# Transposes of the attention probabilities as products with a diagonal matrix of reciprocals, and a rearranged opening

## The chip, the cores and the metric

The kernel runs on one core of one Trainium2 chip. The metric is device time in microseconds (us) of one execution; the median of several is given. Engines work from their own queues, each strictly in the order the program gives it: PE (matrix products), DVE and POOL (elementwise), ACT (copies and functions) and SP (which issues most transfers). They wait for each other through semaphores, written s_... and m_... here.

## The reference

```python
scores = scale * np.matmul(q, k.transpose(0, 1, 3, 2))          # 4 batches, 8 heads, 576 x 64
kth = np.partition(scores, -top_k, axis=-1)[..., -top_k:-top_k + 1]   # top_k = 32
scores = np.where(scores >= kth, scores, -1000000000.0)
attn = np.exp(scores - np.max(scores, axis=-1, keepdims=True))
attn = attn / (np.sum(attn, axis=-1, keepdims=True) + 1e-09)
x = np.matmul(attn, v)                                          # heads side by side: 576 x 512
gate = 1.0 / (1.0 + np.exp(-causal_conv5(x, conv_w)))
x = (gate * (x @ w_val)) @ w_out
u = x + np.real(np.fft.fft(np.fft.fft(x, axis=1), axis=2))
un = (u - u.mean(-1)) / np.sqrt(u.var(-1) + 1e-06)
out = u + np.maximum(un @ w_ch1, 0.0) @ w_ch2
```

## The kernel before

All engines walk through one list of **slots**. Slot s starts the attention tile s (128 query rows against 576 keys of one head; 9 tiles make a pair of heads, 36 a batch, 144 all). The tile t then travels through later slots: scores on PE and their copy `s_sb` on ACT in slot t; the selection of the 32 largest on DVE (`top`, four MAX8 and three MATCH_REPLACE8 for each tile, two tiles at a time) in slots t+1 to t+3; the two bias values on POOL (L917, L918) and the exponent on ACT (`prob`, L655 and L660, with the row sum in `psum_row`) in slot t+5; five 128x128 transposes of `prob` on PE (L455, into `p_t`) and their copy `pT` on ACT (L668) in slot t+6; the product with `v` (L471, `attend`) in slot t+7, for two tiles together, so in five of nine slots.

The softmax is normalised at the end. DVE computes `rinv`, the reciprocal of the row sum (`reciprocal`, L801 and L803); at the end of `attend` two more products (L475) of the broadcast `rinv` with the identity put the reciprocals beside the result; ACT copies both halves to `or_sb` (L677), and POOL multiplies them into `x_new` (L929), which the next stage reads.

From slot 43 on each slot also holds one to three **steps** of the gated layer and the feed-forward layer of the batch before (`val`, `zed`, `seq`, `proj`, `trn`, `ch0`, `ch1`). They are laid out by a table of costs in `steps_by_slot`. A `ch0` or `ch1` step is `hidden` on PE (L574), two copies on ACT (L716, L717), their difference `hid_lo` on POOL (L982) and, one step later, `sums` on PE (L588). In a slot PE does the scores, the transposes, the first step, `attend`, then the other steps. ACT does copy of scores, copy of `pT`, exponent, weight part, first step, output copy, other steps. POOL does the biases, the weight part, the first step, `scale_out` (L929), the other steps. In slots 2 to 33 ACT and POOL also split one weight tile into a high and a low part for each slot (L686 on ACT, then L934 on POOL). After the last attention tile the steps of the fourth batch run alone.

At the start SP issues the loads of q and k of the first pair (first head to `q_raw`, `k_raw`, second head to `z`), then v, the identity, 2.8 MB of tables, two weight tiles, and in slot 0 the q and k of the second pair. ACT takes the high parts of q and k (`high_queries`, `high_keys`), POOL and DVE the low parts (`split_low`). At the ends of slots 0 and 1 ACT takes the high parts of q and k of the next pair.

The products in 32-bit floats show two records each in the trace (a high and a low pass), a transpose one; the f32r products of the scores and of the feed-forward layer show one.

## Time and profile before

| | |
|---|---|
| median of 3 runs | 1178.61 us (1178.06 to 1179.55) |
| profiled execution | 1173.26 us, of which 1171.5 us are its span |
| busy share of the span | PE 88%, DVE 75%, ACT 53%, POOL 34% |
| granted TensorE clock, mean | 0.948 of full speed |

The profiled execution is 5 us below the median. The views used are the busy time by stretches of the span, the timeline (instructions in order of time with the idle time of the engine ahead of each, and who ended it), the groups by line, and the answer by tile. In the timeline, several instructions of one kind that follow each other are one row, with their count after the x; the time of such a row is from the first start to the last end.

### The profile page before, as it was taken

To read this page: it belongs to the slowest core of one execution; us is meant where nothing else is said; L and a number is where in the kernel's file an instruction comes from. 1 tells how busy PE (TensorE), PEld (TensorE's weight loads), DVE (VectorE), ACT (ScalarE), POOL (GpSimd) and SP (SyncE) were. 2 spreads that over 40 slices of the span, in tenths; PEclk is the share of its full clock that TensorE was granted. 3 is DMA by queue.
4 is the path that set the end of the run, shared out by engine and by line. 5 is a ranking of instruction groups with operands and counts; after the bars stand their busy time and mean duration, and the time that the engine had idled before them with its cause. 6 is when DMAs were issued, how large, how long until landed. Compare 5 with 4: busy or idle time off the path is not lost.

```text
span 1171.5 us, 19830 instructions
## 1 busy us (share of the span) xinstructions
PE 1036.1 (88%) x6608; PEld 827.8 (71%) x6608; DVE 872.8 (75%) x1900; ACT 617.6 (53%) x1253; POOL 404.1 (34%) x704
## 2 busy tenths in 40 slices
PE   2776675589988999999989999999889999999998
PEld 1445554466667888866578888875678888648887
DVE  3999999998998897897898987897988960320000
ACT  2676675645466665645466756455565654012211
POOL 1443552223344422332443423233443222233221
PEclk9986566789999999999999999999999999999999
DMA  6755456111256675620367675411367555207974
GB/s 199 228 178 174 156 189 231 32 31 57 68 172 227 246 257 208 205 67 21 112 222 253 251 231 199 145 57 59 134 204 259 201 211 196 99 1 288 343 269 164
DMA packets 81188, 200.37 MB, mean 171 GB/s; under 512 B 8384, under 2 KB 26560, under 8 KB 81088
## 3 DMA queue, kind: packets, MB, share of 16 engines
q1 hardware_dynamic: 81088, 199.11, 50.2%
q8 instruction: 54, 0.88, 0.3%
q14 instruction: 46, 0.38, 0.1%
HBM read 177.58 MB, written 21.50 MB: 170 GB/s over the span
## 4 chain that ended last, share of the span: by engine, by line
PE 38%; issue 26%; DVE 18%; POOL 12%; ACT 3%; SPq 1%; DMA 1%; POOLq 0%; DVEq 0%; ACTq 0%
PE p_m L482 11%; PE p_m L588 10%; PE p_m L574 10%; DVE rest L770 8%; DVE top L776 6%; POOL hid_lo L982 3%; PE p_t L455 2%; PE p_t L471 2%; POOL bias L918 2%; PE p_s L442 2%; POOL bias L917 2%; DVE top L761 1%; ACT prob L655 1%; POOL x_new L929 1%; POOL gate L941 1%
## 5 line engine op out<-in xcount | busy, mean ns | idle before, releaser
L776 DVE MAX8 top<-rest 128x8 f32<-128x576 f32 x432 | 304.6, 746 | 0.0
L770 DVE MATCH_REPLACE8 rest<-top,rest 128x576 f32<-128x576 f32 x288 | 211.7, 743 | 0.0
L982 POOL TENSOR_TENSOR hid_lo<-hid,hid_hi 128x256 fp32r<-128x256 f32 (+1 forms) x128 | 105.0, 820 | 302.5 <-ACT hid_hi L717 302.5
L588 PE MATMUL p_m<-w_st,hid_hi 128*128 128x512 f32 x640 | 202.3, 397 | 1.5 <-POOL hid_lo L982 1.5
L574 PE MATMUL p_m<-un_hi,w_st 128*128 128x320 f32 (+1 forms) x1024 | 165.6, 304 | 13.3 <-ACT hid_hi L717 9.5
L655 ACT ACTIVATE prob<-s_sb,bias 128x576 f32<-128x576 f32 x144 | 111.1, 771 | 104.3 <-POOL bias L918 104.0
L574 PEld LDWEIGHTS p_m<-un_hi,w_st 128*128 128x128 f32 x1024 | 142.8, 189 | 26.4 <-issue 23.4
L455 PE MATMUL p_t<-id_sb,prob 128*128 128x128 f32 x720 | 118.3, 299 | 45.1 <-ACT prob L660 23.7
L471 PE MATMUL p_t<-pT,v_sb 128*64 128x128 f32 (+1 forms) x1600 | 111.8, 293 | 38.2 <-issue 26.1
L648 ACT ACTIVATE s_sb<-p_s 128x576 f32<-128x576 f32 x144 | 93.2, 647 | 96.2 <-PE p_s L442 96.0
L442 PE MATMUL p_s<-k_hi,q_st 128*128 128x512 f32 (+1 forms) x320 | 116.1, 365 | 29.7 <-ACT s_sb L648 19.9
L471 PEld LDWEIGHTS p_t<-pT,v_sb 128*64 128x64 f32 x1600 | 92.2, 153 | 67.1 <-issue 50.7
L588 PEld LDWEIGHTS p_m<-w_st,hid_hi 128*128 128x128 f32 x640 | 113.4, 189 | 20.7 <-POOL hid_lo L982 3.0
L588 PE MATMUL p_m<-w_st,hid_lo 128*128 128x512 f32 x320 | 127.0, 397 | 0.0
L716 ACT ACTIVATE hid<-p_m 128x256 f32<-128x256 f32 (+1 forms) x128 | 51.5, 403 | 139.7 <-PE p_m L574 139.7
L660 ACT ACTIVATE prob<-prob,bias 128x576 f32<-128x576 f32 x144 | 111.8, 776 | 13.1 <-ACT prob L655 0.4
L455 PEld LDWEIGHTS p_t<-id_sb,prob 128*128 128x128 f32 x720 | 82.6, 149 | 50.1 <-ACT prob L660 44.4
L761 DVE MAX8 top<-s_sb 128x8 f32<-128x576 f32 x144 | 101.4, 744 | 11.9 <-ACT s_sb L648 11.9
L668 ACT ACTIVATE pT<-p_t 128x640 f32<-128x640 f32 x144 | 101.4, 704 | 14.8 <-PE p_t L455 14.7
L770 DVE MATCH_REPLACE8 rest<-top,s_sb 128x576 f32<-128x576 f32 x144 | 105.7, 741 | 0.0
L442 PEld LDWEIGHTS p_s<-k_hi,q_st 128*128 128x128 f32 x320 | 66.8, 209 | 53.8 <-issue 29.7
L853 DVE TENSOR_TENSOR u<-p_m,u 128x512 f32<-128x512 f32 (+1 forms) x20 | 12.6, 681 | 112.9 <-PE p_m L588 112.9
(83 smaller groups left out, 1580.1 us busy)
## 6 DMA issues: line engine op xcount, KB each, us to landing
w_st<-w_split SPq DMA_DIRECT2D x256, 512.0 KB, 4.5
w_split<-w_st SPq DMA_DIRECT2D x32, 512.0 KB, 3.0
q_raw<-qT SPq DMA_DIRECT2D x62, 144.0 KB, 2.9
k_raw<-kT SPq DMA_DIRECT2D x62, 144.0 KB, 3.0
u<-w_ch SPq DMA_DIRECT2D x32, 256.0 KB, 3.4
v_sb<-v SPq DMA_DIRECT2D x16, 256.0 KB, 3.6
wslot<-w_val SPq DMA_DIRECT2D x4, 1024.0 KB, 5.3
wslot<-w_out SPq DMA_DIRECT2D x4, 1024.0 KB, 5.3
```

What stands on the lines that cost most here:

```text
L442: mm = pe.matmul(p_s[:, k0:k1], q_st[h][p % 2][:, cols], k[:, k0:k1], start=n == 0, stop=n == len(parts) - 1)
L455: mm = pe.transpose(p_t[:, c * P:c * P + P], prob[t % 3][:, c * P:c * P + P], id_sb[:, :])
L471: pe.matmul(p_o[D * h:D * h + D, 0, 0:n], v_sb[p % 2][:, c, D * h:D * h + D], pT[tt % 3][:, c, c0:c0 + n], start=c == 0, stop=c == NCH - 1 ...
L482: mm = pe.matmul(bank[0:m, c0:c1], a, w, start=k == 0, stop=k == len(lhs) - 1, skip_group_check=True)
L574: mm = pe.matmul(mbank(HIDDEN_BANK[g], n), w1_st[i % NB1][:, w, k, :], x[:, k, at:at + n], start=part + k == 0, stop=part + k == KC + 1)
L588: mm = pe.matmul(mbank(j), h[i % 2][:, P * j:P * j + P], w2_st[i % NB2][:, w, :], start=f == 0 and part == 0, stop=f == FC - 1 and part == 2)
L655: act.activation(prob[t % 3][:, 0:S], s_sb[t % NS][:, :], ACT.Prelu, bias=bias[t % NK][:, 1:2], scale=-BIG, alpha=1.0 / BIG).then_inc(s_dr ...
L660: act.activation(prob[t % 3][:, 0:S], prob[t % 3][:, 0:S], ACT.Exp, bias=bias[t % NK][:, 0:1], scale=-SCALE, accum_out=psum_row[:, t % NK: ...
L761: dve.max(top[tt % NK][:, 0:8], s_sb[tt % NS][:, :]).then_inc(s_chain, 1)
L770: dve.match_replace(rest[tt % 2][:, :], top[tt % NK][:, 8 * n - 8:8 * n], src[:, :], LOWEST).then_inc(s_chain, 1)
L776: found = dve.max(top[tt % NK][:, 8 * n:8 * n + 8], rest[tt % 2][:, :])
L982: pool.tensor_tensor(hid_lo[i % 2][:, 0:WIDTH[g]], hid[:, 0:WIDTH[g]], hid_hi[i % 2][:, 0:WIDTH[g]].bitcast(F32), ALU.subtract).then_inc(m ...
```

## The change

- `normaliser` on POOL takes the place of `reciprocal` on DVE and of `scale_out`. For each tile, in the slot of its exponent and behind the first step, POOL adds to the row sum, raises to the power -1, and multiplies the identity by the result: `norm`, a 128x128 matrix with the reciprocals on its diagonal (two buffers).
- `transpose_p` is a 32-bit product of `prob` with `norm` instead of a transpose with the identity. It waits for `s_norm` instead of `s_exp`.
- `attend` loses its two products with `rinv`; `store_out` on ACT copies 128 columns straight to `x_new`.
- Opening: the four loads of the first head are issued by SP (k) and ACT (q) instead of SP alone; the loads of the second pair come ahead of the tables; the low part of the first k is taken by DVE instead of POOL; and for the second pair the high parts of q and k of the first head are taken at the ends of slots 2 and 3 (before 0 and 1), the low ones at the end of slot 3 (before 2).

```diff
 def transpose_p(t):
-    pe.wait_ge(s_exp, t + 1)
-    if t == 0:
-        pe.wait_ge(s_const, 16)
-    else:
+    pe.wait_ge(s_norm, t + 1)
+    if t:
         pe.wait_ge(s_pT, t)
     if t and unit_due(t + TRANSPOSE - 1):
-        pe.wait_ge(s_or, unit_of(t + TRANSPOSE - 1 - ATTEND) + 1)
+        pe.wait_ge(s_x, unit_of(t + TRANSPOSE - 1 - ATTEND) + 1)
     for c in range(NCH):
-        mm = pe.transpose(p_t[:, c * P:c * P + P], prob[t % 3][:, c * P:c * P + P], id_sb[:, :])
+        mm = pe.matmul(p_t[:, c * P:c * P + P], prob[t % 3][:, c * P:c * P + P], norm[t % 2][:, :],
+                       start=True, stop=True)
...
-    for h, (tt, c0) in enumerate(src):
-        mm = pe.matmul(p_o[D * h:D * h + D, 1, 0:n],
-                       rinv[:, tt % NK:tt % NK + 1].broadcast_to((P, D)),
-                       id_sb[:, c0:c0 + n], start=True, stop=True, skip_group_check=True)
...
-    act.activation(or_sb[n_u % 2][:, :, 0:n], p_o[:, :, 0:n], ACT.Copy).then_inc(s_or, 1)
+    act.activation(x_new[p % NX][:, at:at + n], p_o[:, 0:n], ACT.Copy).then_inc(s_x, 1)
...
-    dve.tensor_scalar(rinv[:, c], psum_row[:, c], EPS_SUM, 2.0, ALU.add, ALU.mult).then_inc(s_radd, 1)
-    dve.wait_ge(s_radd, t // 2 + 1)
-    dve.reciprocal(rinv[:, c], rinv[:, c]).then_inc(s_rinv, 1)
...
-HIGH_Q, HIGH_K, LOW = {0: 0, 4: 1}, {1: 0, 5: 1}, {2: 0, 6: 1}
+HIGH_Q0, HIGH_K0, LOW0 = {2: 0, 5: 1}, {3: 0, 5: 1}, {3: 0, 6: 1}
...
+def normaliser(t):
+    c = slice(t % NK, t % NK + 1)
+    pool.wait_ge(s_exp, t + 1)
+    pool.tensor_scalar(rinv[:, c], psum_row[:, c], EPS_SUM, 2.0, ALU.add, ALU.mult).then_inc(s_radd, 1)
+    pool.wait_ge(s_radd, t + 1)
+    pool.tensor_tensor(rinv[:, c], rinv[:, c], power[:, 1:2], ALU.pow).then_inc(s_rinv, 1)
+    pool.wait_ge(s_rinv, t + 1)
+    if t == 0:
+        pool.wait_ge(s_const, 16)
+    elif t >= 2:
+        pool.wait_ge(s_tr, t - 1)
+    pool.tensor_scalar(norm[t % 2][:, :], id_sb[:, :], rinv[:, c], None, ALU.mult).then_inc(s_norm, 1)
...
-    if unit_due(s):
-        scale_out(s - ATTEND)
+    if due(s, EXPONENT):
+        normaliser(s - EXPONENT)
```

POOL in the first batch, slots 8 and 9, before (`w_st` is the low part of a weight tile):

```order
L917 TENSOR_SCALAR bias<-top 128x1 [waits s_topk]
L918 TENSOR_SCALAR bias<-top 128x1
L934 TENSOR_TENSOR w_st<-u,w_st 128x512 [waits s_whi]
L929 TENSOR_TENSOR x_new<-or_sb 128x128 [waits s_or]
L917 TENSOR_SCALAR bias<-top 128x1 [waits s_topk]
L918 TENSOR_SCALAR bias<-top 128x1
L934 TENSOR_TENSOR w_st<-u,w_st 128x512 [waits s_whi]
```

The same two slots on POOL in the changed kernel:

```order
L916 TENSOR_SCALAR bias<-top 128x1 [waits s_topk]
L917 TENSOR_SCALAR bias<-top 128x1
L935 TENSOR_TENSOR w_st<-u,w_st 128x512 [waits s_whi]
L922 TENSOR_SCALAR rinv<-psum_row 128x1 [waits s_exp]
L924 TENSOR_TENSOR rinv<-rinv,power 128x1 [waits s_radd]
L930 TENSOR_SCALAR norm<-id_sb,rinv 128x128 [waits s_tr,s_rinv]
L916 TENSOR_SCALAR bias<-top 128x1 [waits s_topk]
L917 TENSOR_SCALAR bias<-top 128x1
L935 TENSOR_TENSOR w_st<-u,w_st 128x512 [waits s_whi]
L922 TENSOR_SCALAR rinv<-psum_row 128x1 [waits s_exp]
L924 TENSOR_TENSOR rinv<-rinv,power 128x1 [waits s_radd]
L930 TENSOR_SCALAR norm<-id_sb,rinv 128x128 [waits s_tr,s_rinv]
```

The multiplication of the output is gone, and in every slot three instructions stand behind the weight part that make `norm`.

PE at the end of slot 8 and the start of slot 9, before (one row of L471 stands for ten products of `attend`):

```order
L471 MATMUL p_t<-pT,v_sb 64x128 [waits s_v_in0,s_rinv,s_pT]
L471 MATMUL p_t<-pT,v_sb 64x128 x9
L475 MATMUL p_t<-id_sb,rinv 64x128 x2
L442 MATMUL p_s<-k_hi,q_st 128x512 [waits s_copy,s_lo0]
L442 MATMUL p_s<-k_lo,q_st 128x512
L442 MATMUL p_s<-k_hi,q_st 128x64
L442 MATMUL p_s<-k_lo,q_st 128x64
L455 MATMUL p_t<-id_sb,prob 128x128 [waits s_or,s_pT,s_exp]
L455 MATMUL p_t<-id_sb,prob 128x128 x4
```

The same place on PE in the changed kernel:

```order
L478 MATMUL p_t<-pT,v_sb 64x128 [waits s_v_in0,s_pT]
L478 MATMUL p_t<-pT,v_sb 64x128 x9
L451 MATMUL p_s<-k_hi,q_st 128x512 [waits s_copy,s_lo0]
L451 MATMUL p_s<-k_lo,q_st 128x512
L451 MATMUL p_s<-k_hi,q_st 128x64
L451 MATMUL p_s<-k_lo,q_st 128x64
L462 MATMUL p_t<-norm,prob 128x128 [waits s_x,s_pT,s_norm]
L462 MATMUL p_t<-norm,prob 128x128 x4
```

Two products have left `attend`, and the wait at the head of the transposes is now for POOL's `s_norm`, with `s_x` in the place of `s_or`.

ACT in the opening, slots 0 to 3, before:

```order
L642 ACTIVATE k_hi<-z 128x576 [waits s_qk_in1]
L648 ACTIVATE s_sb<-p_s 128x576 [waits s_qk]
L635 ACTIVATE q_st<-q_raw 128x576 [waits s_qk_in0]
L648 ACTIVATE s_sb<-p_s 128x576 [waits s_qk]
L642 ACTIVATE k_hi<-k_raw 128x576 [waits s_qk_in0]
L648 ACTIVATE s_sb<-p_s 128x576 [waits s_qk]
L686 ACTIVATE w_st<-u 128x512 [waits s_wraw0]
L648 ACTIVATE s_sb<-p_s 128x576 [waits s_qk]
```

The same place on ACT in the changed kernel:

```order
L645 ACTIVATE k_hi<-z 128x576 [waits s_qk_in1]
L651 ACTIVATE s_sb<-p_s 128x576 [waits s_qk] x3
L691 ACTIVATE w_st<-u 128x512 [waits s_wraw0]
L638 ACTIVATE q_st<-q_raw 128x576 [waits s_qk_in0]
L651 ACTIVATE s_sb<-p_s 128x576 [waits s_qk]
L691 ACTIVATE w_st<-u 128x512 [waits s_wraw1]
L645 ACTIVATE k_hi<-k_raw 128x576 [waits s_qk_in0]
```

Three copies of scores now come ahead of the first instruction that waits for a transfer of the second pair or of a weight tile.

## Rows read from the trace of the kernel before

**Rows 1.** Busy time by stretches (us, instructions in brackets), granted clock, transfers.

```profile
core 0: us, PE busy (x) PEld busy (x) DVE busy (x) ACT busy (x) POOL busy (x), PEclk, DMA share, GB/s
40.00:76.00 36.00, 30.20 (x170) 18.61 (x169) 35.90 (x80) 27.18 (x51) 16.29 (x26) 1.00 0.63 195
76.00:220.00 144.00, 92.43 (x581) 76.93 (x579) 143.34 (x305) 96.32 (x181) 56.77 (x95) 0.66 0.52 170
220.00:271.00 51.00, 38.44 (x258) 31.19 (x259) 50.76 (x114) 27.02 (x51) 12.01 (x27) 0.90 0.12 31
271.00:523.00 252.00, 242.35 (x1653) 195.90 (x1651) 219.64 (x475) 149.86 (x309) 92.55 (x167) 1.00 0.52 175
775.00:998.00 223.00, 214.30 (x1459) 171.90 (x1457) 164.30 (x358) 122.43 (x256) 76.19 (x144) 0.98 0.49 171
```

**Rows 2.** Timeline of the opening: start, duration, engine, line, tiles, [idle before].

```profile
16.13 0.60 SPq L324 DMA_DIRECT2D k_raw<-kT  x1
22.47 0.68 ACT L635 ACTIVATE q_st<-q_raw 128x576 fp32r<-128x576 f32 x1 [10.50 <-DMA k_raw<-kT]
23.72 0.76 DVE L761 MAX8 top<-s_sb 128x8 f32<-128x576 f32 x1 [10.96 <-ACT s_sb L648]
39.43 5.40 PE L482 MATMUL p_m<-gv,gate 128*128 128x512 f32 x8
```

**Rows 3.** Timeline, first batch: POOL's weight parts of slots 5, 33; slot 11 whole.

```profile
38.86 1.28 POOL L934 TENSOR_TENSOR w_st<-u,w_st 128x512 fp32r<-128x512 f32 x1 [4.46 <-ACT w_st L686]
...
189.21 1.29 POOL L934 TENSOR_TENSOR w_st<-u,w_st 128x512 fp32r<-128x512 f32 x1 [3.79 <-ACT w_st L686]
...
64.91 0.70 ACT L668 ACTIVATE pT<-p_t 128x640 f32<-128x640 f32 x1
65.52 0.77 ACT L655 ACTIVATE prob<-s_sb,bias 128x576 f32<-128x576 f32 x1
66.32 0.77 ACT L660 ACTIVATE prob<-prob,bias 128x576 f32<-128x576 f32 x1
67.00 0.19 ACT L660 ACTIVATION_READ_ACCUMULATOR prob<-prob,bias 128x1 f32 x1
...
67.79 1.28 POOL L934 TENSOR_TENSOR w_st<-u,w_st 128x512 fp32r<-128x512 f32 x1 [2.64 <-ACT w_st L686]
67.24 0.76 PE L455 MATMUL p_t<-id_sb,prob 128*128 128x128 f32 x5 [1.23 <-ACT prob L660]
```

**Rows 4.** Timeline of POOL at 296 and 302 us: small operations and a 128x128 product.

```profile
296.03 0.22 POOL L958 TENSOR_SCALAR rstd<-mv 128x1 f32<-128x1 f32 x1 [3.15 <-DVE mv L838]
296.34 0.58 POOL L960 TENSOR_TENSOR rstd<-rstd,power 128x1 f32<-128x1 f32 x1
297.00 0.24 POOL L917 TENSOR_SCALAR bias<-top 128x1 f32<-128x1 f32 x1
...
302.80 0.46 POOL L929 TENSOR_TENSOR x_new<-or_sb 128x128 f32<-128x128 f32 x1
```

**Rows 5.** Timeline of PE: transposes, products of several widths, at full clock.

```profile
280.85 3.62 PE L482 MATMUL p_m<-wfeat,gate 128*128 128x257 f32 x16
284.40 1.31 PE L471 MATMUL p_t<-pT,v_sb 128*64 128x128 f32 x20
285.54 0.39 PE L475 MATMUL p_t<-id_sb,rinv 128*64 128x128 f32 x4
285.86 0.50 PE L442 MATMUL p_s<-k_hi,q_st 128*128 128x512 f32 x1
...
641.79 0.77 PE L455 MATMUL p_t<-id_sb,prob 128*128 128x128 f32 x5
642.31 1.19 PE L574 MATMUL p_m<-un_hi,w_st 128*128 128x256 f32 x8
```

**Rows 6.** Timeline of PE: the transposes at the lower clock.

```profile
156.10 1.33 PE L455 MATMUL p_t<-id_sb,prob 128*128 128x128 f32 x5 [1.87 <-ACT prob L660]
```

**Rows 7.** Timeline of POOL and PE around one `ch1` step and one `proj` step.

```profile
704.41 0.88 POOL L982 TENSOR_TENSOR hid_lo<-hid,hid_hi 128x320 fp32r<-128x320 f32 x1 [2.84 <-ACT hid_hi L717]
705.63 0.77 PE L455 MATMUL p_t<-id_sb,prob 128*128 128x128 f32 x5
...
566.09 0.76 PE L455 MATMUL p_t<-id_sb,prob 128*128 128x128 f32 x5
569.33 0.57 POOL L960 TENSOR_TENSOR rstd<-rstd,power 128x1 f32<-128x1 f32 x1
```

**Rows 8.** Groups by line and shape: count, busy us, mean ns.

```profile
L801 DVE TENSOR_SCALAR rinv<-psum_row 128x2 f32<-128x2 f32 x72 | 12.7, 177 | 78.4 <-ACT prob L660 78.4
L803 DVE RECIPROCAL rinv<-rinv 128x2 f32<-128x2 f32 x72 | 11.9, 166 | 2.5
L677 ACT ACTIVATE or_sb<-p_t 128x256 f32<-128x256 f32 x64 | 24.3, 380 | 68.1 <-PE p_t L475 68.1
L907 POOL TENSOR_TENSOR q_st<-q_raw,q_st 64x576 fp32r<-64x576 f32 x16 | 22.6, 1410 | 6.6 <-ACT k_hi L642 6.6
L909 POOL TENSOR_TENSOR k_lo<-k_raw,k_hi 128x576 fp32r<-128x576 f32 x16 | 24.2, 1516 | 0.0
```

**Rows 9.** The page's part on transfers: count, KB each, us to landing.

```profile
u<-w_ch SPq DMA_DIRECT2D x32, 256.0 KB, 3.4
```

99 lines of the change are left out of this document (46 added, 53 removed).

## The prediction

> **What bounds the kernel now.** I read the busy time by stretches first [rows 1]. It shows three regimes. From 40 to 271 us, the attention of the first batch, DVE is busy for 99% of the time (143.34 of 144 us in the middle stretch) while PE has 64% there at a granted clock of 0.66, a mix of its two levels, 1.2 and 2.4 GHz. From 271 to 998 us PE is the bound: 242.35 of 252 us in one batch period at full clock, DVE 87%. From 998 us on the feed-forward steps of the last batch run alone (174 us) and nothing in the change touches them.
>
> The timeline of the opening comes second [rows 2]. The last load of the second pair is issued at 16.13 us and lands at 22.47; ACT waits for it for 10.50 us with the copy of the second tile's scores queued behind, and DVE idles 10.96 us. Third, the timeline of one slot of the first batch [rows 3] shows which steps follow each other between two transposes, and fourth the PE rows [rows 5, 6] give the price of a transpose and of its neighbours.
>
> **What becomes a loop.** Before, the transposes of tile t in slot t+6 waited for the exponent of slot t+5. Now they wait for POOL's `norm`, and POOL makes it only after the weight part of that slot, which itself waits for ACT's weight copy, which stands behind the exponent. The exponent of the next tile stands on ACT behind the copy `pT` of these transposes. So transposes, `pT`, exponent, ACT weight copy, POOL weight part, `norm`, next transposes are one closed chain per slot. Its length, link by link:
>
> - `pT` start to the end of the exponent: 64.91 to 67.19, 2.28 us; from there to the end of POOL's weight part (67.79 + 1.28 = 69.07): 1.88 us [rows 3].
> - `norm`: the trace of before has no such group, its parts have neighbours [rows 4]. The first small operation to the start of the power is 0.31 us (296.03 to 296.34), the power to the next operation 0.54 to 0.66, and a 128x128 product 0.46. Together 1.37 us. The last is one input and a scalar per row instead of two inputs, so 0.24 (a small operation) to 0.46; I take 0.46, since its size is that of the product. Bounds 1.1 to 1.5.
> - transposes to `pT`: 0.80 us in all at full clock now, 1.36 at the lower one [rows 5, 6].
>
> What a product costs instead of a transpose has two ends. Five transposes take 0.52 us from their start to the next group (641.79 to 642.31), 0.104 each. A 32-bit product with 257 columns takes (284.40 - 280.85)/16 = 0.222 us for each of its two records; scaled to 128 columns 0.111, so 0.222 for a product and 1.11 for five. The other end is `attend`: (285.54 - 284.40)/20 = 0.057 a record, 0.57 for five [rows 5]. In `attend` two products of 64 output rows each stand side by side in different halves of the array, here a product fills it, so I take 1.11, that is +0.59 us per tile at full clock. At the lower clock the five take 1.33 in the row, ten records some 2.4, +1.07 (my estimate: 0.21 a record added to the last one's 0.27 doubled).
>
> On its rule about this the Trainium skill ("TensorE: Matmul & The Clock Gate", Terms) says that the transpose mode is four times faster for 32-bit floats. By that a product would be 0.42 us, five 2.08, and the 106 tiles below would add 165 us instead of 63. The row above speaks for about two times.
>
> The chain is then 0.80 + 0.54 (0.59 less overlap at the tail) + 2.28 + 1.88 + 1.37 + 0.04 for the semaphore = 6.9 us at full clock, and 0.56 + 0.55 more = 8.0 at the lower.
>
> **The sum, part by part** (made against the profiled execution, 1173.26 us).
>
> *Opening.* DVE could start its selection some 10.6 us earlier, nearly the 10.96 us. But ACT then waits for the first weight tile, which lands with the tables at about 22 us (now they are all in flight until 22.47), and POOL reaches its first weight parts only then. Its part is done at 22.5 + 0.6 + 1.28 = 24.4, the third weight tile is requested only then and lands 3.4 us later [rows 9], its copy and part end near 30 behind the split of q and k (2.9 [rows 8]); biases, exponent (2.3 with `pT`, 1.6 without) and the part of slot 5 (1.9 [rows 3]) follow: 34 instead of 40.14. **-6** (0 to -11, DVE's whole idle time).
>
> *First batch, slots 5 to 33.* POOL's weight parts end at 38.86 + 1.28 = 40.14 in slot 5 and at 189.21 + 1.29 = 190.50 in slot 33 [rows 3]: 150.4 us for 28 slots, 5.37 each. That is DVE's pace. The chain is longer, so it takes over. The first 7 slots ran at full clock, 7 x 6.9 = 48. For the other 21 I keep the clock of the stretch, 0.66, so a third at full clock: 0.33 x 6.9 + 0.67 x 8.0 = 7.6, times 21 = 160. In three of these slots POOL also splits q and k (1.41 + 1.52 [rows 8]) between `norm` and the next biases, about 1 us each that nothing covers: 3. Together 211 against 150: **+61**. At full clock throughout and with `norm` at 1.1: 28 x 6.6 = 185, +35; at the lower clock throughout with 1.5: +75. What DVE saves (0.177 + 0.166 us for two tiles [rows 8]) buys nothing here, since DVE now waits.
>
> *Slots 34 to 42.* No weight parts, so the chain is 1.9 us shorter, 5.0 to 6.1, against 5.7 now (51 us for nine slots [rows 1]). DVE is caught up by then. **-2** (-7 to +4).
>
> *PE work from slot 43 on.* 106 tiles still have their transposes here: 106 x 0.59 = +63. Each of 60 `attend` groups loses its last products, 285.54 to 285.86 = 0.32 [rows 5]: -19. Together **+44** (-13 with the price of `attend`). PE is 96% busy, so nearly all of it lands on the path; of the 4% idle I let 5 us cover some: **-5**.
>
> *Waits for `norm` from slot 43 on.* In each slot I compared the time at which POOL has done its first step (and ACT its exponent) with the start of the transposes in the next slot, and took as late what is missing to the 1.37 us of `norm`. Two of the pairs are in [rows 7]: after a `ch1` step `hid_lo` ends at 704.41 + 0.88 = 705.29 and the transposes start at 705.63, 0.34 later, so they would be 1.0 us late; after `proj` POOL ends at 569.90 while the transposes had started at 566.09, 5.2 late. In the period from 523 us this gives, for 20 of 36 slots: nine slots with one feed-forward step in front 0.6 to 1.8 each, 10 in all; three slots with `val` 5.6; seven with `seq`, `proj` or `trn` 15.8. That is 31 for a period, 92 for three. PE only hides it where a slot has a second step (late 0 in twelve of these). In the second kind POOL's own date hangs on DVE, which will have more room: after `proj` the true lateness is the chain from PE's last product over DVE's four operations and POOL's two to `norm`, less what PE has to do meanwhile, 2 to 3 us instead of 3 to 5. That takes off 8 a period, 24. POOL's split of q and k behind `norm` adds about 1.2 in two slots a period, 7. Together **+75** (35, if half of it goes into slack, to 110).
>
> *Nothing:* ACT's shorter output copy (0.380 us for 256 columns [rows 8]) and POOL's lost multiplication (0.46 [rows 4]) lie in slack of engines 53% and 34% busy. The tables start some 2 to 3 us later (four transfers stand ahead of them); before, the last transfer of the opening had landed at 22.47 and PE first read them at 39.43 [rows 2].
>
> Sum: -6 + 61 - 2 + 44 - 5 + 75 = +167. The profiled execution would be 1340, and against the median, 1178.6 + 167, **1346 us**.
>
> **The rivals.**
>
> *The waits vanish in the later batches.* If most of the later slots have slack that the single rows don't show, only the first batch's chain and PE's work remain, with 10 us of waits: 1281. For it: POOL is 34% busy. Against it: the hand-over after a lone step has 0.3 us of room and recurs in every period.
>
> *The clock stays up in the first batch.* The granted clock fell to 0.66 where PE had transposes and short products with gaps between. With products instead the stretch could keep 2.4 GHz: 21 x (7.6 - 6.9) = 15 less, 1331. Against it: PE's share per slot falls, as slots get longer. The Trainium skill (same page, Part 4: PE-mode transpose) says that transposes don't count as activity for the clock; that rule is what this case would follow, and no row of before separates it from the gaps.
>
> *A product costs four transposes.* Then 106 x (1.56 - 0.59) = 103 more: 1449.
>
> *`norm` never comes last at all, but the work stays.* Opening and PE's work alone: 1178.6 - 6 + 39 = 1212. Against it stands the closed chain.
>
> *Faster than before.* The mechanism is POOL running ahead: `norm` is ready before PE asks for it in every slot, DVE's pace is kept in the first batch, and a product costs what `attend` shows. Price: -11 in the opening, -6 for DVE's 36 reciprocals and sums (18 x 0.34), -13 on PE: 1149. It decides at the end of POOL's first step: `norm` would have to fit in the 0.34 us of room [rows 7], and in the first batch in less than nothing, since the weight part ends at 69.07, 1.8 us after the transposes started at 67.24 [rows 3]. It is the least likely.
>
> **How the numbers follow.** Forecast 0.62 (own range 1300 to 1395); waits vanish later 0.13; clock 0.12; four times the price 0.04; no wait at all 0.05; faster 0.03; no change 0.01. The range 1270 to 1400 takes in the first three and their bounds and leaves out about 0.15. A measurement of this kernel tells some 0.2% from no change. Faster 0.03, within 0.2% 0.01, slower 0.96.
>
> **What the profile would show.** In the first batch DVE's busy share falls from 99% to some 70 to 75%, its idle time ends with ACT's copies of scores, and POOL's weight parts come 7 to 8 us apart. PE's idle time before the transposes ends with POOL's `norm`, in nearly every slot of the first batch and in about half of the later ones. The group of transposes has 1440 records, ten in a row 1.1 to 1.2 us long. A period of the middle grows from 252 to about 290 us; the part after the last tile stays at 174. Wrong would be: DVE still at 99% in the first batch (no closed chain), a period under 265 (waits were hidden), ten records under 0.7 us (price of `attend`), or a clock near 1.00 between slots 13 and 33.

## The result and the profile after

The changed kernel takes **1422.55 us** (median of 4 executions, 1419.65 to 1426.52), the kernel before 1178.34 beside it. The ratio is 1.208, with a 95% interval of 1.205 to 1.211: 21% slower. The prediction was 1346 with a range of 1270 to 1400. The sign and the two mechanisms (a closed chain in the first batch, more work and waits for PE later) were right, the size was not: 167 us were forecast and 244 came. The largest step that failed is a term that the prediction put at nothing, the lower clock of PE's work behind its waits in the later periods.

The busy time by stretches of the changed kernel: the slots 6 to 33, 34 to 42, and two periods of 36 slots. The stretches end at the starts of the copies `pT`, so that they hold the same slots as those of other kernels below.

```profile
core 0: us, PE busy (x) PEld busy (x) DVE busy (x) ACT busy (x) POOL busy (x), PEclk, DMA share, GB/s
44.00:281.50 237.50, 145.04 (x737) 117.65 (x737) 152.82 (x305) 108.35 (x204) 102.46 (x174) 0.63 0.35 112
281.50:338.70 57.20, 38.95 (x232) 34.22 (x231) 43.23 (x87) 29.85 (x56) 21.86 (x47) 0.68 0.31 97
338.70:641.40 302.70, 269.57 (x1745) 221.06 (x1745) 208.12 (x425) 149.54 (x304) 132.95 (x255) 0.97 0.42 139
641.40:945.10 303.70, 269.55 (x1745) 220.91 (x1745) 213.25 (x436) 149.40 (x304) 133.46 (x255) 0.97 0.42 142
```

The kernel before, in the same slots of the first batch and in its second period:

```profile
core 0: us, PE busy (x) PEld busy (x) DVE busy (x) ACT busy (x) POOL busy (x), PEclk, DMA share, GB/s
40.00:194.00 154.00, 108.56 (x659) 83.77 (x658) 153.38 (x331) 109.25 (x205) 68.30 (x108) 0.72 0.55 176
496.50:748.80 252.30, 243.02 (x1645) 195.42 (x1645) 218.26 (x471) 148.49 (x306) 92.52 (x168) 0.99 0.50 171
```

In the first batch DVE's share has fallen from 99% [rows 1] to 64%, and nothing else has risen to take its place: no engine is the bound there, a chain is. In the periods PE is still busiest, but it is busy for 27 us more and idle for 34 us instead of 9, and its granted clock is 0.97 instead of 0.99.

One turn of the chain in the first batch, from the timelines of PE, ACT and POOL of the changed kernel (columns as in [rows 2]):

```profile
158.27 2.50 PE L462 MATMUL p_t<-norm,prob 128*128 128x128 f32 x10 [1.86 <-POOL norm L930]
160.80 0.71 ACT L671 ACTIVATE pT<-p_t 128x640 f32<-128x640 f32 x1 [3.72 <-PE p_t L462]
161.40 0.77 ACT L658 ACTIVATE prob<-s_sb,bias 128x576 f32<-128x576 f32 x1
162.26 0.78 ACT L663 ACTIVATE prob<-prob,bias 128x576 f32<-128x576 f32 x1
162.94 0.19 ACT L663 ACTIVATION_READ_ACCUMULATOR prob<-prob,bias 128x1 f32 x1
...
163.73 1.26 POOL L935 TENSOR_TENSOR w_st<-u,w_st 128x512 fp32r<-128x512 f32 x1 [4.82 <-ACT w_st L691]
165.08 0.19 POOL L922 TENSOR_SCALAR rinv<-psum_row 128x1 f32<-128x1 f32 x1
165.35 0.57 POOL L924 TENSOR_TENSOR rinv<-rinv,power 128x1 f32<-128x1 f32 x1
166.03 0.63 POOL L930 TENSOR_SCALAR norm<-id_sb,rinv 128x128 f32<-128x128 f32 x1
...
166.71 1.65 PE L462 MATMUL p_t<-norm,prob 128*128 128x128 f32 x6 [5.06 <-POOL norm L930]
```

Every row waits for the one above it. The products take 2.53 us until `pT` starts, `pT` and the exponent 2.33 (to 163.13), the weight copy and the weight part 1.86 (to 164.99), `norm` 1.67 (to 166.66), and 0.05 us later the next products start: 8.44 us. In the stretch 44 to 281.5, 18 of the 28 slots are 8.3 to 8.6 us long; the mean is 8.49.

Two groups of the page: the products and the multiplication that makes `norm` (the last figures are busy us, mean ns, and idle time before with its releaser).

```profile
L462 PE MATMUL p_t<-norm,prob 128*128 128x128 f32 x1440 | 239.3, 323 | 201.5 <-POOL norm L930 201.5
...
L930 POOL TENSOR_SCALAR norm<-id_sb,rinv 128x128 f32<-128x128 f32 x144 | 94.2, 654 | 14.9
```

PE waits 201.5 us for `norm` in the whole span. In the period from 641.4 to 945.1 it is 31.7 us in 20 waits, from the view of waits of that stretch:

```profile
PE p_t L462 <- POOL norm L930: 31.7, 20, 4.8
```

The table compares stages of the profiled executions (before, this one is 5 us below its median) by the starts of the `pT` copies of tiles 0, 28, 37, 73, 109 and 143 in the timelines, in us (forecast: the prediction's terms, those of slots 43 on divided by three).

| stage | before | after | more | forecast |
|---|---|---|---|---|
| until slot 6 | 39.8 | 44.0 | +4.2 | -6 |
| slots 6 to 33 | 153.8 | 237.6 | +83.8 | +61 |
| slots 34 to 42 | 48.8 | 57.2 | +8.4 | -2 |
| slots 43 to 78 | 254.1 | 302.7 | +48.6 | +38 |
| slots 79 to 114 | 252.3 | 303.7 | +51.4 | +38 |
| slots 115 to 148 | 235.3 | 284.6 | +49.3 | +38 |
| the rest | 187.4 | 188.1 | +0.7 | 0 |
| span | 1171.5 | 1417.8 | +246.3 | +167 |

### The profile page after: what moved, and what is told of

Same layout as the page of the kernel before. It is cut to its first block, busy times and chain, and to the rows that moved or that the text cites. A ratio compares the mean times of both kernels' runs of the same rounds, so it can differ in the third digit from the quotient of the medians.

```text
span 1417.8 us, 20820 instructions
## 1 busy us (share of the span) xinstructions
PE 1163.5 (82%) x7008; PEld 948.0 (67%) x7008; DVE 855.7 (60%) x1758; ACT 619.6 (44%) x1253; POOL 571.0 (40%) x1055
## 4 chain that ended last, share of the span: by engine, by line
PE 55%; POOL 19%; ACT 10%; issue 10%; DVE 4%; DMA 1%; SPq 1%; POOLq 0%; ACTq 0%; DVEq 0%
PE p_t L462 15%; PE p_m L485 14%; PE p_m L577 10%; PE p_m L591 10%; ACT prob L658 4%; POOL norm L930 4%; POOL rinv L924 4%; PE p_t L478 3%; POOL w_st L935 2%; PE p_s L451 2%; POOL hid_lo L983 2%; ACT prob L663 2%; POOL rinv L922 2%; ACT w_st L691 1%; DVE rest L777 1%
## 5 line engine op out<-in xcount | busy, mean ns | idle before, releaser
L462 PE MATMUL p_t<-norm,prob 128*128 128x128 f32 x1440 | 239.3, 323 | 201.5 <-POOL norm L930 201.5
L462 PEld LDWEIGHTS p_t<-norm,prob 128*128 128x128 f32 x1440 | 209.4, 227 | 213.1 <-POOL norm L930 213.0
L671 ACT ACTIVATE pT<-p_t 128x640 f32<-128x640 f32 x144 | 101.4, 704 | 303.7 <-PE p_t L462 303.7
L768 DVE MAX8 top<-s_sb 128x8 f32<-128x576 f32 x144 | 105.1, 749 | 184.0 <-ACT s_sb L651 184.0
L577 PE MATMUL p_m<-un_hi,w_st 128*128 128x320 f32 (+1 forms) x1024 | 173.1, 313 | 7.6 <-issue 3.8
L577 PEld LDWEIGHTS p_m<-un_hi,w_st 128*128 128x128 f32 x1024 | 150.1, 198 | 19.7 <-issue 16.5
L591 PEld LDWEIGHTS p_m<-w_st,hid_hi 128*128 128x128 f32 x640 | 114.2, 190 | 18.9 <-POOL hid_lo L983 1.1
L930 POOL TENSOR_SCALAR norm<-id_sb,rinv 128x128 f32<-128x128 f32 x144 | 94.2, 654 | 14.9
```

Source lines behind the costliest of these rows:

```text
L462: mm = pe.matmul(p_t[:, c * P:c * P + P], prob[t % 3][:, c * P:c * P + P], norm[t % 2][:, :], start=True, stop=True)
L577: mm = pe.matmul(mbank(HIDDEN_BANK[g], n), w1_st[i % NB1][:, w, k, :], x[:, k, at:at + n], start=part + k == 0, stop=part + k == KC + 1)
L591: mm = pe.matmul(mbank(j), h[i % 2][:, P * j:P * j + P], w2_st[i % NB2][:, w, :], start=f == 0 and part == 0, stop=f == FC - 1 and part == 2)
L930: pool.tensor_scalar(norm[t % 2][:, :], id_sb[:, :], rinv[:, c], None, ALU.mult).then_inc(s_norm, 1)
```

## Experiments

My theory from these rows: the time goes into a closed chain over PE, ACT and POOL, whose price is set by `norm` standing behind late work on POOL; a second, smaller part is PE's own work; and the clock adds to both, because PE pauses before each group of products. The rivals: the products themselves are the cost, or POOL's operations are too long. The stages of all kernels, measured as above, by tiles (in `later`, `ahead`, `shift` and `relief`, whose transposes come one slot later, the same tiles lie one slot further on):

| kernel | slots 6-33 | 34-42 | 43-78 | 79-114 | 115-148 | clock, whole span |
|---|---|---|---|---|---|---|
| before | 153.8 | 48.8 | 254.1 | 252.3 | 235.3 | 0.948 |
| after | 237.6 | 57.2 | 302.7 | 303.7 | 284.6 | 0.902 |
| `opening` | 151.7 | 49.3 | 255.1 | 252.2 | 235.3 | 0.948 |
| `product` | 155.7 | 48.2 | 271.5 | 266.7 | 249.0 | 0.967 |
| `wait` | 209.7 | 50.6 | 288.1 | 298.5 | 272.6 | 0.886 |
| `later` | 182.7 | 47.4 | 276.0 | 279.7 | 255.7 | 0.939 |
| `ahead` | 145.5 | 39.6 | 278.1 | 266.5 | 244.4 | 0.972 |
| `early` | 181.3 | 58.2 | 273.4 | 272.7 | 252.5 | 0.951 |
| `one` | 208.1 | 47.1 | 280.6 | 283.3 | 264.8 | 0.930 |
| `warm` | 227.2 | 57.9 | 302.8 | 303.8 | 284.5 | 0.933 |
| `shift` | 146.8 | 49.8 | 271.6 | 260.2 | 241.0 | 0.939 |
| `relief` | 144.2 | 47.7 | 266.7 | 261.7 | 239.5 | 0.937 |
| `lighten` | 146.1 | 48.2 | 251.8 | 252.0 | 233.3 | 0.955 |

### The opening alone

```diff
-                load_qk(0, 0)
+                for half in range(2):
+                    sp.dma_start(k_raw[D * half:D * half + D, :], kT[0, 0]).then_inc(s_qk_in[0], 16)
...
+                load_qk(1, 0)
...
+HIGH_Q0, HIGH_K0, LOW0 = {2: 0, 5: 1}, {3: 0, 5: 1}, {3: 0, 6: 1}
```

> The kernel before with the opening of the change alone; transposes, reciprocals and output as before. Theory (DVE sets the pace of the first batch, so what it no longer idles at the start is gained): the second tile's selection starts at 13.4 us instead of 23.7, later stalls at the first weight tile give some 2 us back, so 8 us less, 1170 us (0.993). Rival (the wait of 7.6 us that ACT now has for the first weight tile moves the stall and keeps it): within 3 us of before.

Measured: 1171.59 us, ratio 0.9953 (0.9936 to 0.9969), 5.7 us less. The total is near the expected 1170, though the gain is not where I put it: in its trace the copy `pT` of tile 0 starts at 39.03 instead of 39.78, not 8 us earlier. The two profiled executions differ by only 1.2 us (spans of 1170.3 and 1171.5), so the traces don't show where the other 4.5 of the 5.7 us lie. Where the gain of the opening was lost shows in the opening of the changed kernel, whose part up to the exponent is the same (timelines of DVE, ACT, SP's queue, POOL and PE):

```profile
13.37 0.76 DVE L768 MAX8 top<-s_sb 128x8 f32<-128x576 f32 x1 [1.59 <-ACT s_sb L651]
...
32.68 0.43 SPq L351 DMA_DIRECT2D u<-w_ch  x1
...
36.84 0.63 ACT L691 ACTIVATE w_st<-u 128x512 fp32r<-128x512 f32 x1 [2.47 <-DMA u<-w_ch]
...
37.55 1.27 POOL L935 TENSOR_TENSOR w_st<-u,w_st 128x512 fp32r<-128x512 f32 x1 [4.89 <-ACT w_st L691]
...
41.45 2.50 PE L462 MATMUL p_t<-norm,prob 128*128 128x128 f32 x10 [8.73 <-POOL norm L930]
```

DVE selects from the second tile at 13.37 instead of 23.72 [rows 2], 10.4 us earlier. But the weight part of slot 5 ends at 38.82 instead of 40.14, only 1.3 us earlier: its tile is requested at 32.68, because SP had four loads and a store that waits for POOL ahead of it. In the changed kernel the first products then wait for `norm` until 41.45.

### The product alone

```diff
-        mm = pe.transpose(p_t[:, c * P:c * P + P], prob[t % 3][:, c * P:c * P + P], id_sb[:, :])
+        mm = pe.matmul(p_t[:, c * P:c * P + P], prob[t % 3][:, c * P:c * P + P], id_sb[:, :],
+                       start=True, stop=True)
```

> The kernel before with the five transposes of each tile written as 32-bit products with the identity, same waits, same result. It prices the product alone. Theory (a product costs two records of 0.11 us, nearly all of it on the path from slot 43 on, nothing in the first batch where DVE is the bound): 106 tiles x 0.6 = 64 us more, 1242 us, clock of the first batch not above 0.7. Rival 1 (a product costs four transposes): 165 us more, 1343. Rival 2 (products count as activity for the clock where transposes don't): granted clock of 76 to 220 us near 1.0 instead of 0.66.

Measured: 1223.54 us, ratio 1.040 (1.038 to 1.042), 46 us more. The price of a product, from its timeline and its stretches:

```profile
606.67 1.36 PE L455 MATMUL p_t<-id_sb,prob 128*128 128x128 f32 x10
607.79 1.18 PE L575 MATMUL p_m<-un_hi,w_st 128*128 128x256 f32 x8
```

```profile
43.00:198.60 155.60, 113.53 (x798) 92.70 (x797) 154.77 (x330) 109.36 (x205) 70.00 (x106) 0.84 0.53 169
518.20:784.90 266.70, 261.94 (x1826) 216.55 (x1825) 220.09 (x472) 151.11 (x304) 91.10 (x167) 1.00 0.48 161
```

Ten records take 1.12 us to the next group, against 0.52 for five transposes [rows 5]: +0.60, where the prediction took 0.59. The rival of four times the price is refuted. A period grows by 14.4 us: PE is busy 18.9 longer (36 tiles x 0.52), and 4.5 of that falls into idle time. In the first batch, where DVE is the bound, the products cost nothing (1.9 us in 28 slots). And the granted clock there is 0.84 instead of 0.72, with the same pace. In slots 34 to 42 it is 0.79 in both kernels. How much it varies by itself shows in `opening`, whose PE work is the same as before: 0.76 and 0.68 in these two stretches.

### The wait alone

```diff
-        mm = pe.matmul(p_t[:, c * P:c * P + P], prob[t % 3][:, c * P:c * P + P], norm[t % 2][:, :],
-                       start=True, stop=True)
+        mm = pe.transpose(p_t[:, c * P:c * P + P], prob[t % 3][:, c * P:c * P + P], id_sb[:, :])
```

(against the changed kernel; the transposes still wait for `norm`, but don't use it)

> The changed kernel with the five products turned back into transposes with the identity, which still wait for POOL's norm; the normalisation is left out of the result. It prices the closed chain alone. Theory (the chain over POOL makes most of the loss, and its length is the sum of its links): in the first batch about 7.2 us a slot at the lower clock instead of 8.45, 50 us more than before from slot 6 to slot 34; in each later period 20 to 30 us of waits for norm; together 1178 - 8 + 50 + 80 - 19 = 1280 us. Rival (the product makes the loss, the wait only takes what PE idles anyway): under 1220 us.

Measured: 1350.46 us, ratio 1.148 (1.145 to 1.150). That is 173 us more than before and 70 over what I expected, so the wait is dearer than forecast. Its stretches, slots 6 to 33 and the second period:

```profile
42.40:252.10 209.70, 117.95 (x597) 88.18 (x597) 152.29 (x307) 108.03 (x205) 101.79 (x174) 0.60 0.39 125
590.80:889.30 298.50, 257.02 (x1565) 204.10 (x1564) 215.56 (x435) 148.79 (x305) 136.49 (x255) 0.93 0.43 144
```

In the period this kernel has *less* work on PE than the one before (the products with `rinv` are gone, 1565 records instead of 1645), and PE is yet busy for 257.0 us instead of 243.0: the same work runs at a granted clock of 0.93 instead of 0.99. With products in the place of the transposes and the same waits the clock is 0.97, and the period only 5 us longer (303.7). So in this period the two parts don't add up: with the waits in place, the product's 14 us are for the greater part offset by a better clock. The other two periods don't repeat this. There the clock of `wait` is 0.96 and 0.94, that of the changed kernel 0.97 and 0.96, and the products cost 14.6 and 12.0 us (302.7 against 288.1, 284.6 against 272.6). In the first batch, where the chain is closed, the products do cost: 237.6 against 209.7, 1.0 us a slot.

### One slot more between the exponent and the products

```diff
-SELECT, EXPONENT, TRANSPOSE, ATTEND = 1, 5, 6, 7
+SELECT, EXPONENT, TRANSPOSE, ATTEND = 1, 5, 7, 8
```

> The changed kernel with the transposes and the product with v one slot later (7 and 8 slots behind the scores instead of 6 and 7); same operations, same result. The exponent then no longer stands behind the transposes of the tile before it, so the chain is open. Theory (it is the chain, not POOL's load): slots of the first batch back to 5.4 us, no waits for norm above a few us a period, what stays is PE's work: 1178 - 8 + 5 for one more slot + 3 x 18 = 1229 us. Rival (POOL is too busy with 1.7 us more a slot): first batch still above 7 us a slot, over 1320 us.

Measured: 1273.84 us, ratio 1.082 (1.080 to 1.084). The chain over PE is open, 149 us come back, but the first batch needs 182.7 us, 6.5 a slot, and not DVE's 5.4. The timelines of POOL and ACT show what closes instead:

```profile
124.25 0.30 POOL L917 TENSOR_SCALAR bias<-top 128x1 f32<-128x1 f32 x1
124.58 0.78 ACT L658 ACTIVATE prob<-s_sb,bias 128x576 f32<-128x576 f32 x1 [1.12 <-POOL bias L917]
...
126.92 1.27 POOL L935 TENSOR_TENSOR w_st<-u,w_st 128x512 fp32r<-128x512 f32 x1 [2.37 <-ACT w_st L691]
...
129.23 0.63 POOL L930 TENSOR_SCALAR norm<-id_sb,rinv 128x128 f32<-128x128 f32 x1
...
130.26 0.30 POOL L917 TENSOR_SCALAR bias<-top 128x1 f32<-128x1 f32 x1
```

Biases, exponent, weight copy, weight part, `norm`, next biases: 6.0 us in this turn, all on ACT and POOL; the copies `pT` come 3.3 to 8.7 us apart in that stretch, so it is not closed in each of them, and that this loop sets the mean of 6.5 is shown only by the next experiment. `norm` stands at the end of POOL's slot and ahead of the next biases, so it lengthens this loop too. I had not seen it; before, it was 1.7 us shorter and hidden behind DVE.

### And `norm` right behind the biases

```diff
                     if due(s, EXPONENT):
                         biases(s - EXPONENT)
+                    if due(s, EXPONENT + 1):
+                        normaliser(s - EXPONENT - 1)
```

(on top of the last edit, with the old call removed)

> As the kernel with the transposes one slot later, and POOL makes norm of the tile before directly behind the biases, where it no longer waits for ACT's exponent and runs beside it. Theory (with the chain over PE open, the first batch hangs on a second chain, biases, exponent, weight copy, weight part, norm, next biases, 6.0 us; without norm in it 4.4): first batch back to DVE's pace, 5.4 to 5.6 us a slot, 1274 - 28 x 1.0 = 1246, and less in the later periods, where the step behind norm starts sooner: 1220 to 1246 us. Rival (POOL's load, not its place in the chain): first batch stays at 6.5 us a slot, 1270 us.

Measured: 1209.07 us, ratio 1.027 (1.025 to 1.029).

```profile
43.80:189.30 145.50, 104.61 (x734) 86.73 (x734) 145.36 (x296) 105.56 (x203) 104.74 (x179) 0.85 0.60 194
507.00:773.50 266.50, 257.95 (x1746) 212.49 (x1746) 212.20 (x435) 148.85 (x305) 133.64 (x255) 1.00 0.48 162
```

DVE is the bound again (145.36 of 145.5 us), and the second period is that of the product alone (266.5 against 266.7; the first is 6.5 us longer, the third 4.6 shorter). It issues the same operations as the changed kernel, POOL's among them, and is 213 us faster. It is 31 us slower than the kernel before, 48 if its gain of 17 us in slots 6 to 42 is left aside. So POOL's load and the products together explain at most some 50 of the 244 us: the rest is where `norm` stands and the slot of room behind it, which this run changes together. The second row also bears on the price of the clock. The changed kernel does the same work in its period in 269.55 us instead of 257.95, 11.6 us more, at 0.97 instead of 1.00. Not all of it is the clock: `early` below has the slots of the changed kernel and a clock of 1.00, and its PE is busy for 260.01 us, 2.1 more than here.

### `norm` ahead of the weight part and the first step

```diff
+                    if due(s, EXPONENT):
+                        normaliser(s - EXPONENT)
                     if part_due(s) is not None:
                         split_weights(part_due(s))
```

(transposes in their old slot, the old call removed)

> The changed kernel with norm made on POOL ahead of the weight part and of the first step, transposes in their slot. Theory (the chain stays closed but loses POOL's weight part or step): first batch 8.45 - 1.87 = 6.6 us a slot at the lower clock, 28 x 1.9 = 52 us less, and most of the 32 us of waits in each later period gone: 1422 - 52 - 3 x 25 = 1295 us. Rival (POOL's order does not matter, only its load): within 20 us of 1422.

Measured: 1265.16 us, ratio 1.074 (1.072 to 1.076), 30 less than expected. In the first batch the chain is still closed, without the weight part: 6.5 us a slot, 2.0 less than before that edit, about the 1.86 of that link. In the second period, from its stretches and its waits:

```profile
551.80:824.50 272.70, 260.01 (x1746) 213.24 (x1745) 216.06 (x435) 149.60 (x305) 135.46 (x255) 1.00 0.47 158
```

```profile
PE p_t L462 <- POOL norm L930: 6.7, 7, 2.1
```

The waits for `norm` fall from 31.7 to 6.7 us, 25 less, but the period is 31 shorter: PE's idle time falls by 21.5 us in all, and with the clock back at 1.00 PE is busy for **9.5 us** less. This is what I had missed in my expectation as in the prediction: a microsecond of waiting removed here brings 1.2 back.

### `norm` from one operation

```diff
-                    pool.tensor_scalar(rinv[:, c], psum_row[:, c], EPS_SUM, 2.0, ALU.add, ALU.mult).then_inc(s_radd, 1)
-                    pool.wait_ge(s_radd, t + 1)
-                    pool.tensor_tensor(rinv[:, c], rinv[:, c], power[:, 1:2], ALU.pow).then_inc(s_rinv, 1)
-                    pool.wait_ge(s_rinv, t + 1)
...
-                    pool.tensor_scalar(norm[t % 2][:, :], id_sb[:, :], rinv[:, c], None, ALU.mult).then_inc(s_norm, 1)
+                    pool.tensor_scalar(norm[t % 2][:, :], id_sb[:, :], psum_row[:, c], None, ALU.mult).then_inc(s_norm, 1)
```

(the kernel leaves out the reciprocal, so its output is not normalised; ACT's wait for the sum becomes a wait for `norm`)

> The changed kernel with the sum and the power left out: norm is the identity times the row sum in one operation, so the result is not normalised. 0.95 us less on POOL for each tile. Theory (each microsecond of norm lies on the path wherever PE waits for it: all 37 slots of the first batch, 19 of 36 in each period): 37 x 0.95 + 3 x 19 x 0.95 x 0.8 = 35 + 43, 1422 - 78 = 1344 us. Rival (the semaphore hand-overs and the order make the loss, not the length): under 30 us less.

Measured: 1317.04 us, ratio 1.118 (1.116 to 1.120). The chain row by row loses 165.08 to 166.03, 0.95 us; the slots 6 to 33 lose 29.5 / 28 = 1.05. In the first batch the chain's length is thus the time, link for link. The second period loses 20.4: its waits for `norm` fall from 31.7 us in 20 places to 15.0 in 11, and PE is busy for 264.49 us instead of 269.55, at 0.98. The last part, 5.1 us, is as in the last experiment, and with the other periods it is a reason why the gain of 106 us was above the expected 79.

### Filler products against the clock

```diff
+                    if 14 <= s < 42:
+                        fill(s, 5)
                     if due(s, TRANSPOSE):
                         transpose_p(s - TRANSPOSE)
```

(five products of 128x512 into an unused part of `p_m`, between the scores and the transposes, in the changed kernel)

> The changed kernel with five more 512-column products into an unused PSUM bank in each of the slots 14 to 41, between the scores and the wait for norm; same result. They lie in PE's idle time (2.2 to 5.3 us a slot there). Theory (the lower clock lengthens the chain by the product's 1.1 us): granted clock of that stretch from 0.63 to 0.95 or more, slots of 7.4 instead of 8.45 us, 28 us less, 1394 us. Rival (the clock is not what sets the slots): the same 1422 us or more, with the clock up.

Measured: 1408.65 us, ratio 1.196 (1.193 to 1.198). The mean clock of slots 6 to 33 rises from 0.63 to 0.79, yet they take 227.2 us instead of 237.6, only 10.4 less; all other stages are unchanged. Two groups of its products for the transposes:

```profile
157.57 1.38 PE L468 MATMUL p_t<-norm,prob 128*128 128x128 f32 x10 [0.84 <-POOL norm L938]
...
164.91 2.13 PE L468 MATMUL p_t<-norm,prob 128*128 128x128 f32 x10 [4.13 <-POOL norm L938]
```

After a wait of 0.84 us they take 1.38 us, as at 2.4 GHz; after one of 4.13 us they take 2.13, nearer to the 2.50 of the lower level. Of the 21 groups of the slots 14 to 34, 12 take 1.27 to 1.52 us, four 1.98 to 2.13 and five 2.50; in the changed kernel only two of the same 21 take less than 2.50. Ten groups more at the higher level, 1.1 us each, are about what was gained. The seven groups behind a wait of 4.1 us all take 2.07 us or more: the fillers stand ahead of the wait, and part of the higher clock goes to work that nobody waits for. So the mean clock of a stretch is not the clock of the instructions that matter in it.

### Which parts of the change are worth keeping

`ahead` was faster than the kernel before in slots 6 to 42 (185.1 us against 202.6). I asked whether that comes from the free slot or from the work taken off DVE. `shift` has the new opening and the slots 7 and 8, with transposes and `attend` as before:

```diff
-SELECT, EXPONENT, RECIP, TRANSPOSE, ATTEND = 1, 5, 6, 6, 7
+SELECT, EXPONENT, RECIP, TRANSPOSE, ATTEND = 1, 5, 6, 7, 8
```

> The kernel before with the new opening, and transposes and attend one slot later (7, 8), DVE's reciprocals where they were. Theory (the gain of the run ahead over before in slots 6 to 43, 185.1 against 202.6 us, comes from the free slot between exponent and transposes, not from anything in the change): 28 slots of the first batch stay at DVE's pace, 150 to 153 us, the nine slots 34 to 42 fall from 49 to 40 us, later periods stay at 252. Sum from the opening run's 1171.6: -9, and +2 for the one slot more at the end: 1165 (1160 to 1169). Rival (the gain of ahead came from DVE's lost reciprocals and PE's shorter attend): the nine slots stay at 47 to 49 us, 1172 to 1175.

`relief` also moves the reciprocals to POOL, as powers, right behind the biases:

```diff
-                    dve.reciprocal(rinv[:, c], rinv[:, c]).then_inc(s_rinv, 1)
...
+                    if due(s, EXPONENT + 1):
+                        reciprocal(s - EXPONENT - 1)
```

> As shift, and the reciprocals made by POOL right behind the biases (sum and power, 128x1 each, 0.9 us a tile with their gap) instead of by DVE; transposes with the identity and the products of rinv in attend as before. Theory (DVE is the bound of the first batch, so 14 x 0.34 us of reciprocals off it are worth their time, and POOL's additions are hidden because they wait for nothing late): first 28 slots 146 to 148 us, 5 less than shift, later periods 252: 1159 (1153 to 1164). Rival (0.9 us more on POOL between the biases and the weight part makes weight parts and steps late): 28 slots as in shift or longer and later periods 254 to 258, 1166 to 1180.

Measured: `shift` 1204.02 us, ratio 1.023 (1.022 to 1.025), `relief` 1192.92, ratio 1.013 (1.012 to 1.014). Both are slower than before, and outside of what theory and rival gave. The first 28 slots did get faster (146.8 and 144.2), but the nine after them hardly (49.8, 47.7), and the later periods lost 16, 8 and 6 us in `shift`. At the start of the steps PE waits once for 11.33 us, for a `pT` that stands on ACT behind `gate`, and `gate` waits for DVE (its timeline):

```profile
255.89 0.68 ACT L696 ACTIVATE gate<-gate 128x576 f32<-128x576 f32 x1 [13.92 <-DVE gate L827]
...
257.00 0.70 ACT L674 ACTIVATE pT<-p_t 128x640 f32<-128x640 f32 x1
257.75 2.40 PE L477 MATMUL p_t<-pT,v_sb 128*64 128x128 f32 x20 [11.33 <-ACT pT L674]
```

In `opening` the same `gate` starts at 256.98, but ACT has copied that tile's `pT` at 245.72 and waits only 2.40 us. So the free slot is not free: PE's product with `v` now needs a `pT` from behind that wait. This one wait is most of the 16 us; the 8 and 6 us of the later periods I did not follow. What the two have told apart is the work on DVE: `relief` is 11 us faster than `shift`. `lighten` keeps the old slots, with the new opening and the reciprocals on POOL:

> The kernel before with the new opening and with the reciprocals made by POOL right behind the biases instead of by DVE, transposes and attend in their old slots (6, 7). Theory (the run relief gained 11 us on the run shift because DVE, the bound of the first batch, loses 0.17 us a tile, and this carries over; its other losses came from the slot moved): slots 6 to 43 in 194 to 197 us against 200.9 of the run opening, later periods at 252 to 254, 1165 (1161 to 1169). Rival (0.9 us more on POOL between the biases and the weight part or the first step shows in the closed part of the old order, exponent, transposes, exponent, where nothing has a free slot): first batch as in opening, later periods 254 to 258, 1172 to 1182.

Measured: **1163.86 us**, ratio 0.988 (0.986 to 0.991), as expected and faster than both kernels, the one before by 1.2%.

```profile
39.00:190.00 151.00, 101.56 (x660) 78.36 (x658) 149.68 (x301) 111.39 (x210) 94.82 (x169) 0.76 0.56 180
...
496.00:748.00 252.00, 242.84 (x1646) 195.58 (x1645) 214.01 (x435) 148.60 (x305) 121.14 (x239) 0.99 0.50 171
```

The slots 6 to 42 take 194.3 us instead of 200.9 in `opening`, DVE being the bound in both, and POOL's 29 us more in a period cost nothing. Nobody waits at once for the reciprocals here: they are read in the next slot.

## Why the prediction was wrong, point by point

**Direction and mechanisms: right.** The closed chain exists, link by link as described, and DVE waits in the first batch. The last part is unchanged, PE's waits in a period end with `norm`, and the chance of 0.96 for slower was on the right side. The last two rivals, no wait at all and faster, fell at once, as did four times the price.

**From slot 43 on: work and idle time near the forecast, a third term missing.** The runs divide what each period lost. The reference for PE's work at full clock is `early`, which has the changed kernel's operations in the same slots and whose clock is back at 0.99 to 1.00; PE's busy times in the three periods are 242.79, 243.02 and 225.52 us before, 261.64, 260.01 and 240.36 in `early`, 269.57, 269.55 and 249.52 in the changed kernel.

| slots | more | work (`early` - before) | clock (after - `early`) | idle time (after - before) |
|---|---|---|---|---|
| 43 to 78 | 48.6 | 18.9 | 7.9 | 21.8 |
| 79 to 114 | 51.4 | 17.0 | 9.5 | 24.9 |
| 115 to 148 | 49.3 | 14.8 | 9.2 | 25.3 |
| sum | 149.3 | 50.7 | 26.6 | 72.0 |
| forecast | 114 | 44 | nothing | 75 - 5 |

**The step that failed most: PE's work from slot 43 on was priced at full clock.** The prediction did so because the rows of before show it there [rows 1], and never asked what its own 20 waits a period would do to that. Some 27 us in three periods are work at a lower clock, a term that it put at nothing. `early` ties them to the waits: with 25 us of waits less, the clock is back at 1.00.

**The waits themselves: right by luck in part.** The idle time came out as forecast, but not the waits for `norm`. They are 30.6, 31.7 and 33.2 us in the three periods, 95.5 in all, where the term was 75. Of these 20 us more, `norm` being 0.3 us longer than the forecast had it (below) makes up some 17, in 58 waits. The idle time rose by less than the waits for `norm`, because other waits of before went away. In the second period, before and then changed:

```profile
PE p_t L455 <- ACT or_sb L677: 3.9, 3, 1.9
PE p_m L574 <- ACT hid_hi L717: 2.7, 4, 1.8
...
PE p_m L577 <- ACT hid_hi L722: 0.8, 2, 0.6
```

**The first batch, "For the other 21 I keep the clock of the stretch, 0.66": failed.** It also gave the first seven slots full clock because they had it before. In the changed kernel 22 of the 28 groups of products take 2.50 us and only six 1.36 to 1.44. The forecast amounts to 14 groups at the lower clock, so eight too few: 8 x 1.1 = 9 us. In this batch every group behind a wait of 4.6 us or more takes 2.50.

**`norm` at 1.37 us: mis-sized.** It measured 1.67 from the end of the weight part. The multiplication of the identity with one scalar a row takes 0.654 us, where I took the 0.46 of a product of two 128x128 tiles as an upper end. 0.3 x 28 = 8 us in the first batch. The products at the lower clock take until `pT` 2.53 us, where the terms of the chain had 2.45, and `pT` and the exponent 2.33 for 2.28: another 0.13 us a slot, 4 us.

**Two delays that the forecast of the first batch did not have.** In the slots of tiles 3, 5 and 7 not `norm` but PE came last. One of them, from the timelines of PE and POOL:

```profile
59.41 5.02 PE L485 MATMUL p_m<-gv,gate 128*128 128x512 f32 x8
64.36 1.31 PE L478 MATMUL p_t<-pT,v_sb 128*64 128x128 f32 x20
64.81 0.63 POOL L930 TENSOR_SCALAR norm<-id_sb,rinv 128x128 f32<-128x128 f32 x1
66.30 1.36 PE L462 MATMUL p_t<-norm,prob 128*128 128x128 f32 x10
```

`norm` is ready at 65.44, but PE is behind with eight products of the setup and `attend`, so these slots are 8.05 to 8.52 us long although their products run at full clock: 3 us in all. And in three slots the first two operations of `norm` took 0.67 and 0.96 us instead of 0.19 and 0.57, each time while DVE made the low parts of q and k:

```profile
113.89 0.82 DVE L797 TENSOR_TENSOR q_st<-q_raw,q_st 64x512 fp32r<-64x512 f32 x2 [3.97 <-ACT k_hi L645]
114.10 0.67 POOL L922 TENSOR_SCALAR rinv<-psum_row 128x1 f32<-128x1 f32 x1
114.64 0.74 DVE L799 TENSOR_TENSOR k_lo<-k_raw,k_hi 128x576 fp32r<-128x576 f32 x1
114.85 0.96 POOL L924 TENSOR_TENSOR rinv<-rinv,power 128x1 f32<-128x1 f32 x1
```

That is 0.87 us each, 2.6 in all; no run separates its cause. Clock, `norm`, products and these two delays come to 26 of the 26.6 us by which the 211 us of the term fell short of 237.6.

**Slots 34 to 42, -2: wrong sign.** The chain without the weight part is 8.44 - 1.86 = 6.6 at the lower clock, where the bound was 6.1. Nine slots took 57.2 us, 6.4 each. It is the same two errors, and a reading: the 51 us that the prediction set against these slots are the stretch from 220 to 271 us [rows 1], but they lie from 193.6 to 242.4 and took 48.8.

**Opening, -6: +4.2.** I let the weight part of slot 5 end at 34 us, from the arrival of the third weight tile; it is the fourth that slot 5 needs, and SP requests it only at 32.68. The part ended at 38.82. Then the first `norm` cost 2.6 us behind it, on a path where the transposes before had started at once (38.31).

**The rival "the clock stays up": half right.** With products in the place of transposes the clock was higher in two pairs: 0.84 against 0.72 at the same pace in the first batch, and 0.97 against 0.93 with the same waits in the second period. In slots 34 to 42 it was the same, 0.79 (`product` and before). The Trainium skill ("TensorE: Matmul & The Clock Gate", Part 4: PE-mode transpose) says that transposes don't count as busy time for the clock in the way that other products do. The two pairs agree with it but don't show it, since a product also keeps PE at work for twice as many records; no run here tells the kind of instruction from its length. And the rival's result, a first batch at full clock, did not come (0.63): the waits outweigh what the products give.

## What to carry to other kernels

When an edit puts a wait ahead of a group of products, its price is not the wait alone but also the clock of the work behind it; here 25 us of waits took 9.5 us more from a period in which the engine was otherwise at full clock. On an in-order queue the place of an operation can weigh more than its length: three operations on POOL at the end of a slot made the kernel 213 us slower than the same three right behind the biases of the next slot with one slot more of room. Either alone gave back 157 us (`early`, another place) or 149 (`later`, more room). And look at who waits for the result of an operation that is moved off the bounding engine: the one part of this change that paid beside the opening was the reciprocal, whose result is read only in the next slot.
